# Attention, four experts and a SoLU layer: the experts' first layer as seven block products

## The chip, the cores and the metric

The kernel runs on one core of one Trainium2 chip. The time is the device time of one execution in microseconds, the median of several runs. TensorE (PE in the rows; PEld is its weight load), VectorE (DVE), ScalarE (ACT), GpSimd (POOL) and SyncE (SP, which issues most transfers) work side by side and wait for one another through semaphores.

## What is computed

```python
a = attention(q, k, v)            # 2 x 8 heads, 768 rows, 64 wide: 8 first keys and a band of 96
x = a as rows                     # 1536 x 512
p = probs / (probs.sum(-1) + 1e-9)
for e in range(4):                # w1[e] 512 x 1024, w2[e] 1024 x 512
    h = np.maximum(x @ w1[e], 0.0)
    out += p[:, e:e+1] * (h @ w2[e])
h = out @ w_in                    # 512 x 1024
solu = h * softmax(h)
ln = (solu - mean) / sqrt(var + 1e-6) * g_ln
return ln @ w_out                 # 1536 x 512
```

Everything is float32. The matmuls of the experts and of the last layer run in the format fp32r, in which TensorE takes one pass, but with fewer bits; so each operand is split into `hi` (the rounded value) and `lo` (what is left), and a product is three matmuls into one sum: hi·hi, hi·lo, lo·hi. ScalarE and GpSimd make the `hi` parts by a copy into fp32r, VectorE and GpSimd the `lo` parts by a subtraction.

## The kernel before

The program has three stages.

**Attention.** Heads go two at a time, eight pairs, each in three steps of 128 x 2 rows; `j` counts rounds of two pairs, six steps b = 0 to 5. In one step TensorE does `scores(b)`, `turn(b-1)` (transposes of the exponentials) and `values(b-2)`; VectorE adds the bias and takes row maxima (`add_bias`, L1034), ScalarE the exponentials (L830); both copy transposes out of PSUM (L840, L1043). After a pair VectorE normalises it (L1050 to L1056), TensorE transposes it (`turn_pair`, L623), ScalarE writes `xT_hi` (L846) and VectorE `xT_lo` (L1064). GpSimd meanwhile builds the values' windows (`copy_windows`, L480), the biases (`scale_bias`) and expert 0's first-layer weights (`split_w1`, L455 and L457).

**Experts.** The 1536 tokens go in three groups of 512, for four experts: `STEPS` = 12 steps n of eight chunks c of 128 hidden columns. `hidden(n, c)` (L569) computes one chunk, transposed, for 512 tokens: 4 slices of x by 3 matmuls, w stationary, x streaming 512 columns. ScalarE's `relu_hi` (L825) and VectorE's `relu_lo` (L1014) turn the bank in PSUM into h_hi and h_lo. `mix(n, c)` (L690) multiplies four token tiles of them, stationary, with the chunk's rows of w2, 512 columns streaming, into four banks `y_ps` that collect all eight chunks. `hidden` is three chunks ahead of `mix`:

```python
with pe.Fori(0, STEPS - 1) as n:
    for c in range(FC):
        hidden(n, c + AHEAD) ...   # or hidden(n + 1, c + AHEAD - FC)
        mix(n, c)
```

At the end of a step VectorE's `add_up` (L1172, L1174) adds the four banks, weighted with the expert's probability, to `acc`. GpSimd splits the next expert's weights chunk by chunk as the old ones come free (L461, L463).

**Last layer.** Twelve tiles s of 128 tokens: VectorE stages rows of `acc` (`stage`, L1195), TensorE transposes them (`turn_x`, L701) and multiplies with w_in (`up`, L743); `norm` on VectorE (L1219 to L1248) with ScalarE's exponential and one small power on GpSimd (L553); then `turn_ln` (L755) and `down` (L765) with w_out, which GpSimd has scaled by the gain (L542) and split. w_in's `hi` part is ScalarE's (L911) and its `lo` part VectorE's (L1257).

Each engine has its own program; the order of work is written out by hand, and is what the loops give.

## Time and profile before

| what | value |
|---|---|
| median of 3 runs (lowest, highest) | 793.17 us (793.15, 794.11) |
| the profiled execution | 793.0 us |
| its span, first to last instruction | 791.1 us |
| TensorE busy, matmuls | 786.6 us, 3838 |
| VectorE, ScalarE, GpSimd busy | 263.6, 164.2, 169.0 us |
| moved by DMA | 36.98 MB |

1.9 us of the profiled execution lie outside its span. The page's first part gives each engine's busy time, its second the span in 40 slices; a matmul's busy time in a row runs from its start to the modelled end of its pipeline, so that neighbours overlap, and how long one holds TensorE is read from starts, or from the chain of waits, which counts each piece up to the next one. A weight load overlaps with the matmul before it.

### The profile page before, as it was taken

How to read it: one execution, taken by the hardware profiler on the slowest of the kernel's cores; microseconds unless marked ns; L12 is line 12 of the kernel's file. 1: busy time of each engine (PE TensorE's matmuls, PEld its weight loads, DVE VectorE, ACT ScalarE, POOL GpSimd, SP SyncE). 2: the span in 40 equal slices, each digit the busy share in tenths (PEclk: the TensorE clock that was granted, in tenths of full speed). 3: DMA queues.
4: the chain of work that ended last, by engine and by line, in shares of the span. 5: the costliest groups of instructions: out<-in, count | busy, mean ns of one | idle time of the engine just before them, and what ended most of it. 6: DMA issues, size and time to landing. Idle time of an engine off the chain costs nothing.

```text
span 791.1 us, 11238 instructions
## 1 busy us (share of the span) xinstructions
PE 786.6 (99%) x3838; PEld 642.1 (81%) x3838; DVE 263.6 (33%) x586; ACT 164.2 (21%) x301; POOL 169.0 (21%) x221
## 2 busy tenths in 40 slices
PE   9999999999999999999999999999999999999998
PEld 8888888888888888888888888888888888888886
DVE  5676621211212121211212121211214268565653
ACT  4666511110101010101010111101011213222222
POOL 5334530000562000066000016620001320000000
PEclk9999999999999999999999999999999999999999
DMA  9744730000005000000500000130000000000001
GB/s 264 197 129 138 232 108 1 0 0 0 0 0 212 0 0 0 0 0 0 212 0 0 0 0 0 62 150 0 0 0 1 0 1 14 27 13 27 14 27 40
DMA packets 34133, 36.98 MB, mean 47 GB/s; under 512 B 14145, under 2 KB 25409, under 8 KB 34113
## 3 DMA queue, kind: packets, MB, share of 16 engines
q1 hardware_dynamic: 32000, 34.64, 13.8%
q10 hardware_dynamic: 2112, 2.10, 0.8%
q8 instruction: 10, 0.16, 0.1%
q14 instruction: 11, 0.08, 0.0%
HBM read 33.59 MB, written 3.15 MB: 46 GB/s over the span
## 4 chain that ended last, share of the span: by engine, by line
PE 95%; issue 4%; DVE 0%; POOL 0%; ACT 0%; POOLq 0%
PE y_ps L690 34%; PE h_ps L569 34%; PE out_ps L765 7%; PE h_ps L743 6%; PE o_ps L613 5%; PE s_ps L586 3%; PE pT_ps L596 3%; PE lnT_ps L755 1%; PE h_ps L765 1%; PE xt_ps L623 1%; PE o_ps L707 1%; PE xr_ps L701 0%; PE o_ps L630 0%; POOL stats L553 0%; DVE ln_lo L1205 0%
## 5 line engine op out<-in xcount | busy, mean ns | idle before, releaser
L1014 DVE SCALAR_TENSOR_TENSOR h_lo<-h_ps,h_hi 128x512 fp32r<-128x512 f32 x96 | 66.4, 692 | 403.7 <-ACT h_hi L825 403.7
L825 ACT ACTIVATE h_hi<-h_ps 128x512 fp32r<-128x512 f32 x96 | 57.5, 599 | 467.8 <-PE h_ps L569 467.8
L690 PE MATMUL y_ps<-w_hi,h_hi 128*128 128x512 f32 x384 | 153.2, 399 | 0.0
L690 PE MATMUL y_ps<-w_hi,h_lo 128*128 128x512 f32 x384 | 152.0, 396 | 0.0
L569 PE MATMUL h_ps<-xT_lo,w_hi 128*128 (+1 forms) x384 | 151.9, 396 | 0.0
L569 PE MATMUL h_ps<-xT_hi,w_hi 128*128 (+1 forms) x384 | 151.9, 396 | 0.0
L690 PE MATMUL y_ps<-w_lo,h_hi 128*128 128x512 f32 x384 | 151.7, 395 | 0.0
L569 PE MATMUL h_ps<-xT_hi,w_lo 128*128 (+1 forms) x384 | 151.5, 395 | 0.0
L690 PEld LDWEIGHTS y_ps<-w_hi,h_lo 128*128 128x128 f32 x384 | 72.5, 189 | 18.5
L569 PEld LDWEIGHTS h_ps<-xT_hi,w_hi 128*128 128x128 f32 x384 | 72.1, 188 | 17.8
L690 PEld LDWEIGHTS y_ps<-w_lo,h_hi 128*128 128x128 f32 x384 | 72.1, 188 | 17.4
L569 PEld LDWEIGHTS h_ps<-xT_hi,w_lo 128*128 128x128 f32 x384 | 72.1, 188 | 17.4
L569 PEld LDWEIGHTS h_ps<-xT_lo,w_hi 128*128 128x128 f32 x384 | 72.2, 188 | 17.0
L690 PEld LDWEIGHTS y_ps<-w_hi,h_hi 128*128 128x128 f32 x384 | 72.1, 188 | 16.7
L455 POOL CAST w_hi<-w_raw 128x512 fp32r<-128x512 f32 (+1 forms) x32 | 19.6, 612 | 228.1 <-PE h_ps L569 224.8
L461 POOL CAST w_hi<-w_raw 128x512 fp32r<-128x512 f32 x40 | 24.5, 612 | 188.2 <-issue 95.5
L463 POOL TENSOR_TENSOR w_lo<-w_raw,w_hi 128x512 fp32r<-128x512 f32 x40 | 51.9, 1298 | 3.2
L830 ACT ACTIVATE neg_s<-neg_s,row 128x256 f32<-128x256 f32 (+1 forms) x96 | 42.4, 482 | 26.1 <-DVE row L1034 25.9
L457 POOL TENSOR_TENSOR w_lo<-w_raw,w_hi 128x512 fp32r<-128x512 f32 (+1 forms) x32 | 41.4, 1293 | 2.9 <-POOL w_hi L455 0.7
L613 PE MATMUL o_ps<-v_sb,pT 128*128 128x65 f32 x352 | 42.0, 271 | 0.0
L1034 DVE CUSTOM_DVE_ANT_0 neg_s<-s_ps,bias 128x256 f32<-128x256 f32 (+1 forms) x96 | 34.4, 399 | 21.1 <-PE s_ps L586 18.8
L613 PEld LDWEIGHTS o_ps<-v_sb,pT 128*128 128x128 f32 x352 | 41.3, 192 | 0.1
(98 smaller groups left out, 771.0 us busy)
## 6 DMA issues: line engine op xcount, KB each, us to landing
w_raw<-in_w SPq DMA_DIRECT2D x7, 2048.0 KB, 9.8
qk<-in_qkW SPq DMA_DIRECT2D x24, 256.0 KB, 3.9
...
```

What stands on the lines that cost most here:

```text
L457: nc.gpsimd.tensor_tensor(lo, part, f32(hi), ALU.subtract).then_inc(w1_ready, 1)
L461: nc.gpsimd.tensor_copy(w2_hi[:, c], w2_raw[:, c]).then_inc(w2_hi_ready, 1)
L463: nc.gpsimd.tensor_tensor(w2_lo[:, c], w2_raw[:, c], f32(w2_hi[:, c]), ALU.subtract).then_inc(w2_ready, 1)
L569: mm = nc.tensor.matmul(h_ps[c % H_RING][:, :], w[:, c, k, :], x[:, k, cols], start=(k == 0 and x is xT_hi and w is w1_hi), stop=(k == KC ...
L613: mm = nc.tensor.matmul(o_ps[:, m, i * DV:(i + 1) * DV], pT[:, c % 2, e, (2 * m + half) * P:(2 * m + half + 1) * P], v_sb[:, p, m, at, :], ...
L690: mm = nc.tensor.matmul(y_ps[t][:, :], h[:, c % H_RING, tok], w[:, c, :], start=(c == 0 and h is h_hi and w is w2_hi), stop=(c == FC - 1 a ...
L743: mm = nc.tensor.matmul(h2_ps[m][:, b * HALF:(b + 1) * HALF], x[:, m, k, :], w[:, b * FC // 2:(b + 1) * FC // 2, k, :], start=(k == 0 and ...
L765: mm = nc.tensor.matmul(out_at(s), x[:, m, c, :], w[:, c, :], start=(c == 0 and x is ln_hi and w is w2_hi), stop=(c == FC - 1 and x is ln_lo))
L825: nc.scalar.activation(h_hi[:, c % H_RING, :], h_ps[c % H_RING][:, :], ACT.Relu).then_inc(hhi_ready, 1)
L830: nc.scalar.activation(tile, tile, ACT.Exp, bias=row[:, b // STEPS_PAIR, m, i:i + 1], scale=-1.0).then_inc(exp_ready, 1)
L1014: nc.vector.scalar_tensor_tensor(h_lo[:, c % H_RING, :], h_ps[c % H_RING][:, :], 0.0, f32(h_hi[:, c % H_RING, :]), ALU.max, ALU.subtract). ...
L1034: nc.vector.tensor_tensor_reduce(o, s, c, -SCALE, 3e38, ALU.add, ALU.min, row[:, b // STEPS_PAIR, m, i:i + 1]).then_inc(biased, 1)
```

## The change

The product of one weight block and x is done by Strassen's algorithm, in the form with 15 additions. A step is now 2 chunks (256 hidden columns) of one expert for one batch of 768 tokens. Both are halved three times over: the contraction of 512 in pairs of 128-slices, the 256 hidden columns in two chunks, the 768 tokens in two halves of `NB` = 384. Eight block products of 2 slices each become seven, on seven blocks of weights and seven of x, of which four each are sums of others:

- `ws[slot]`: the seven weight blocks, hi and lo, of a group g of two chunks (16 groups, two slots). GpSimd makes them: `weigh_sums` and `weigh_parts`; `split_w2` splits the group's two chunks of w2.
- `xs`: the seven blocks of x for both batches, made once, in the attention stage. VectorE makes the sums (`even_sums`, `odd_sums`, `odd_rest`), ScalarE the hi parts (`even_hi`, `odd_hi`, `sum_hi`), GpSimd the lo parts of the four sums (`x_lo`).
- `product(s, n, ...)` on TensorE: two slices by three matmuls of 384 columns into one of four banks `p_ps`; seven of them a step, in the order 1, 2, 6, 7, 5, 3, 4, in 16 x 2 = 32 steps s.
- ScalarE copies product 1 to SBUF (`keep`); seven additions of VectorE on 384 columns combine the products into four blocks of h in SBUF (`first_block` to `lower_block`); `relu_hi` and `relu_lo` split each into `hs`, reading it from SBUF.
- `mix(s, t, ...)`: six token tiles a step, each the sum over the step's two chunks only (6 matmuls of 512 columns), in one of three banks; `add_up` adds each of them to `acc`, six times a step.

The mixes of a step lie between the products of the next one. Weights come in transfers of 512 KB a group instead of 2048 KB an expert. w_in and w_out are loaded near the end, and GpSimd alone splits both. The large tensors are laid out anew in SBUF; attention and last layer compute as before. The cut diff:

```diff
-    GT = 4
-    GW = GT * P
-    NG = T // GW
-    STEPS = E * NG
+    NB = S // 2
+    SETS = 7
+    BLOCKS = 4
+    GROUPS = E * FC // 2
+    STEPS = GROUPS * B
+    TILES = QB
+    Y_BANKS = 3
+    ORDER = (1, 2, 6, 7, 5, 3, 4)
+    LAST = STEPS - 1
...
+            def load_weights(g):
+
+                e, q, slot = g // (FC // 2), g % (FC // 2), g % 2
+                sp.wait_ge(w1_ready, g - 1)
+                sp.dma_start(raw[:, slot, :].rearrange("p (k f) -> p k f", k=KC),
+                             w1[e].rearrange("(k p) f -> p k f", p=P)[:, :, 2 * P * q:2 * P * (q + 1)]
+                             ).then_inc(w1_loaded[slot], 16)
+                sp.wait_ge(w2_ready, g - 1)
+                sp.dma_start(raw[:, 2 + slot, :].rearrange("p (f n) -> p f n", f=2),
+                             w2[e].rearrange("(c p) n -> p c n", p=P)[:, 2 * q:2 * q + 2, :]
+                             ).then_inc(w2_loaded[slot], 16)
...
+                nc.gpsimd.tensor_tensor(sum_[:, 4], part(0, 1, slot), part(1, 1, slot), ALU.add).then_inc(w1_step, 1)
+                nc.gpsimd.tensor_tensor(sum_[:, 6], part(0, 0, slot), part(0, 1, slot), ALU.subtract).then_inc(w1_step, 1)
...
+                nc.gpsimd.tensor_copy(hi[:, 3:7], sum_[:, 3:7]).then_inc(w1_step, 1)
...
+                nc.gpsimd.tensor_tensor(lo[:, 3:7], sum_[:, 3:7], f32(hi[:, 3:7]), ALU.subtract).then_inc(w1_ready, 1)
...
+            def x_lo(j):
+
+                pool.wait_ge(xs_sum, START + 6 * j + 5)
+                for n, i in enumerate((5, 6, 4, 2)):
+                    pool.wait_ge(xs_hi, START + 7 * j + 3 + n + 1)
+                    pool.sem_inc(pool_waited, 1)
+                    nc.gpsimd.tensor_tensor(xs[:, j, 0, i], xs_sum_sb[:, j, 0, i], f32(xs[:, j, 1, i]), ALU.subtract
+                                            ).then_inc(xs_lo, 1)
...
+            with pool.Fori(1, GROUPS // 2) as a:
+                for slot in range(2):
+                    weigh_sums(2 * a + slot, slot)
+                    weigh_parts(2 * a + slot, slot)
+                    split_w2(2 * a + slot, slot)
+
+            pool.wait_ge(win_loaded, 16)
+            pool.wait_ge(p_done, SETS * LAST)
             for c in range(FC):
-                split_w2(0, c)
-            with pool.Fori(1, E) as e:
-                pool.wait_ge(w1_loaded, FIRST + 16 * e)
-                pool.wait_ge(w2_loaded, 16 * e + 16)
-                for c in range(FC):
-
-                    pool.wait_ge(h_ready, FC * NG * e - FC + c + 1)
-                    split_w1(e, c)
-                    pool.wait_ge(h_used, H_RING + FC * NG * e - FC + c + 1)
-                    split_w2(e, c)
-
-            pool.wait_ge(w2_loaded, 16 * E + 16)
+                part_c = raw[:, :, c * P:(c + 1) * P]
+                pool.sem_inc(pool_waited, 1)
+                nc.gpsimd.tensor_copy(win_hi[:, c], part_c).then_inc(win_step, 1)
+                pool.wait_ge(win_step, c + 1)
+                pool.sem_inc(pool_waited, 1)
+                nc.gpsimd.tensor_tensor(win_lo[:, c], part_c, f32(win_hi[:, c]), ALU.subtract).then_inc(win_ready, 1)
...
-            def hidden(n, c, chunks=range(KC)):
...
-                for k in chunks:
-                    for w, x in ((w1_hi, xT_hi), (w1_hi, xT_lo), (w1_lo, xT_hi)):
-                        mm = nc.tensor.matmul(h_ps[c % H_RING][:, :], w[:, c, k, :], x[:, k, cols],
-                                              start=(k == 0 and x is xT_hi and w is w1_hi),
...
+            def product(s, n, i, g):
+
...
+                if n == 1:
+                    pe.wait_ge(w1_ready, g + 1)
+                    at_least(pe, p_sum, SETS * s - 4)
+                if n == 2:
+                    at_least(pe, p_sum, SETS * s - 2)
+                if n == 6:
+                    at_least(pe, p_sum, SETS * s - 1)
+                if n == 7:
+                    at_least(pe, p_sum, SETS * s)
+                if n == 5:
+                    pe.wait_ge(p_kept, s + 1)
+                if n == 3:
+                    pe.wait_ge(p_sum, SETS * s + 1)
+                if n == 4:
+                    pe.wait_ge(p_sum, SETS * s + 2)
...
+                for kk in range(2):
+                    for w, x in ((1, 1), (1, 0), (0, 1)):
+                        mm = nc.tensor.matmul(bank, ws[slot][:, w, part, kk, :], xs[:, 2 * bt + kk, x, part, :],
+                                              start=(kk == 0 and w == 1 and x == 1),
+                                              stop=(kk == 1 and w == 0))
+                mm.then_inc(p_done, 1)
+
+            def mix(s, t, slot, bt, g):
+
+                if t == 0:
+                    pe.wait_ge(w2_ready, g + 1)
+                    pe.wait_ge(h_split, BLOCKS * s + BLOCKS)
+                at_least(pe, acc_written, TILES * s + t + 1 - Y_BANKS)
+                tok = slice((t % 3) * P, (t % 3 + 1) * P)
+                for f in range(2):
+                    b = 2 * f + t // 3
+                    for h, w in ((1, 1), (1, 0), (0, 1)):
+                        mm = nc.tensor.matmul(y_ps[t % Y_BANKS][:, :], hs[bt][:, h, b, tok], w2s[slot][:, w, f, :],
+                                              start=(f == 0 and h == 1 and w == 1), stop=(f == 1 and h == 0))
+                mm.then_inc(y_done, 1)
...
-                pe.wait_ge(x_ready, START + HP)
-                hidden(0, 0)
+                pe.wait_ge(xs_sum, START + 12)
+                pe.wait_ge(xs_lo, START + 8)
+                product(0, 1, 0, 0)
+                product(0, 2, 0, 0)
                 values(OUTER, -1)
-                hidden(0, 1)
+                product(0, 6, 0, 0)
+                product(0, 7, 0, 0)
                 turn_pair(OUTER, -1)
-                hidden(0, 2)
+                for n in (5, 3, 4):
+                    product(0, n, 0, 0)
+
...
-            with pe.Fori(0, STEPS - 1) as n:
-                for c in range(FC):
-                    if c + AHEAD < FC:
-                        hidden(n, c + AHEAD)
-                    else:
-                        hidden(n + 1, c + AHEAD - FC)
-                    if c == 0:
-                        pe.wait_ge(x_ready, START + R)
-                    mix(n, c)
...
+            def step(a, i):
+
+                s, g, last = 4 * a + i, 2 * a + i // 2, 4 * a + i - 1
+                last_slot, last_bt, last_g = (i - 1) // 2 % 2, (i - 1) % 2, 2 * a + (i - 1) // 2
+                new = isinstance(a, int) and s == 1
+                if new:
+                    pe.wait_ge(xs_sum, START + 19)
+                product(s, 1, i, g)
+                if new:
+                    pe.wait_ge(xs_sum, START + 24)
+                product(s, 2, i, g)
+                mix(last, 0, last_slot, last_bt, last_g)
+                if new:
+                    pe.wait_ge(xs_lo, START + 13)
...
+                product(s, 7, i, g)
...
+                product(s, 5, i, g)
...
+            def relu_hi(s, b, bt):
+
+                act.wait_ge(p_sum, SETS * s + {0: 1, 3: 4, 1: 6, 2: 7}[b])
+                nc.scalar.activation(hs[bt][:, 1, b], hs_sum[bt][:, 0, b], ACT.Relu).then_inc(hhi_ready, 1)
...
-            def relu_lo(n, c):
-                dve.wait_ge(hhi_ready, FC * n + c + 1)
-                nc.vector.scalar_tensor_tensor(h_lo[:, c % H_RING, :], h_ps[c % H_RING][:, :], 0.0,
-                                               f32(h_hi[:, c % H_RING, :]), ALU.max, ALU.subtract
...
+            def first_block(s, i):
+
+                dve.wait_ge(p_done, SETS * s + 2)
+                dve.wait_ge(p_kept, s + 1)
+                at_least(dve, y_done, TILES * (s - 1))
+                nc.vector.tensor_tensor(hs_sum[i % 2][:, 0, 0], p_bank(i, 2), kept[:, 0, :], ALU.add).then_inc(p_sum, 1)
...
+            def last_block(s, i):
+                dve.wait_ge(p_done, SETS * s + 5)
+                dve.wait_ge(p_sum, SETS * s + 3)
+                nc.vector.tensor_tensor(hs_sum[i % 2][:, 0, 3], p_bank(i, 5), kept[:, 2, :], ALU.add).then_inc(p_sum, 1)
...
+
+            def lower_block(s, i):
+                dve.wait_ge(p_done, SETS * s + 7)
+                nc.vector.tensor_tensor(hs_sum[i % 2][:, 0, 2], p_bank(i, 4), kept[:, 2, :], ALU.add).then_inc(p_sum, 1)
...
+            def relu_lo(s, b, bt):
+
+                dve.wait_ge(hhi_ready, BLOCKS * s + {0: 1, 3: 2, 1: 3, 2: 4}[b])
+                nc.vector.scalar_tensor_tensor(hs[bt][:, 0, b], hs_sum[bt][:, 0, b], 0.0, f32(hs[bt][:, 1, b]), ALU.max, ALU.subtract
                                                ).then_inc(h_split, 1)
...
+            def halve(a, i):
+
...
+                first_block(s, i)
+                add_up(s - 1, 0, 1 - bt, expert, first)
+                relu_lo(s, 0, bt)
+                second_sum(s, i)
+                third_sum(s, i)
+                add_up(s - 1, 1, 1 - bt, expert, first)
+                last_block(s, i)
+                fourth_sum(s, i)
+                add_up(s - 1, 2, 1 - bt, expert, first)
+                relu_lo(s, 3, bt)
+                right_block(s, i)
+                add_up(s - 1, 3, 1 - bt, expert, first)
+                relu_lo(s, 1, bt)
+                lower_block(s, i)
+                add_up(s - 1, 4, 1 - bt, expert, first)
+                relu_lo(s, 2, bt)
+                add_up(s - 1, 5, 1 - bt, expert, first)
```

On TensorE in the expert stage, the loop's body before; `h_ps` is a chunk's bank, `y_ps` a token tile's, rows without a tile prepare waits:

```order
L569 REGISTER_ALU
L569 MATMUL h_ps<-xT_lo,w_hi 128x512
L569 MATMUL h_ps<-xT_hi,w_lo 128x512
L682 REGISTER_ALU
L683 REGISTER_ALU
L687 ISA
L690 MATMUL y_ps<-w_hi,h_hi 128x512
L690 MATMUL y_ps<-w_lo,h_hi 128x512
L690 MATMUL y_ps<-w_hi,h_lo 128x512
```

and of the change, at the start of the loop's body (`p_ps` a product's bank, L48 and L702 the counters for semaphores):

```order
L48 ISA
L693 MATMUL p_ps<-xs,ws 128x384 x6
L48 REGISTER_ALU
L693 MATMUL p_ps<-xs,ws 128x384 x6
L702 ISA
L48 ISA
L708 MATMUL y_ps<-w2s,hs 128x512 x6
L48 REGISTER_ALU
L693 MATMUL p_ps<-xs,ws 128x384 x12
L48 REGISTER_ALU
L708 MATMUL y_ps<-w2s,hs 128x512 x6
```

Twelve matmuls of 512 columns in a chunk have become six of 384 in a product, and `mix` of the step before stands behind products 2, 7, 5, 3 and twice behind 4.

On VectorE where attention ends, before (`x_pair` is the last pair normalised, `xT_lo` its part of x):

```order
L1043 COPY pT<-pT_ps 128x512
L1064 TENSOR_TENSOR xT_lo<-xt_ps,xT_hi 128x768
L1014 SCALAR_TENSOR_TENSOR h_lo<-h_ps,h_hi 128x512
L1050 TENSOR_SCALAR sums<-o_ps 128x12
L1052 RECIPROCAL sums<-sums 128x12
L1056 TENSOR_TENSOR x_pair<-o_ps,sums 128x2x6x64
L1014 SCALAR_TENSOR_TENSOR h_lo<-h_ps,h_hi 128x512
L1064 TENSOR_TENSOR xT_lo<-xt_ps,xT_hi 128x768
```

and of the change, from the third sum of step 0 on (L1223; `kept` and `hs_sum` are sums of products, `hs` the lo part of h, `xs` and `xs_sum` blocks of x):

```order
L1223 TENSOR_TENSOR kept<-p_ps,kept 128x384
L1316 TENSOR_TENSOR xs_sum<-xt_ps,xs_sum 128x384
L1317 TENSOR_TENSOR xs_sum<-xt_ps,xs_sum 128x384
L1228 TENSOR_TENSOR hs_sum<-p_ps,kept 128x384
L1323 TENSOR_TENSOR xs_sum<-xt_ps,xs_sum 128x384
L1324 TENSOR_TENSOR xs<-xt_ps,xs 128x2x384
L1231 TENSOR_TENSOR hs_sum<-p_ps,kept 128x384
L1246 SCALAR_TENSOR_TENSOR hs<-hs_sum,hs 128x384
L1236 TENSOR_TENSOR hs_sum<-p_ps,hs_sum 128x384
L1246 SCALAR_TENSOR_TENSOR hs<-hs_sum,hs 128x384
L1241 TENSOR_TENSOR hs_sum<-p_ps,kept 128x384
L1246 SCALAR_TENSOR_TENSOR hs<-hs_sum,hs 128x384
```

The x of the last pair is now four sums and one subtraction, between the additions of step 0's products, and all of step 0's four `relu_lo` (L1246) stand here.

## Rows read from the trace of the kernel before

**Rows 1.** The page: TensorE busy, and its granted clock in 40 slices.
```profile
PE 786.6 (99%) x3838; PEld 642.1 (81%) x3838; DVE 263.6 (33%) x586; ACT 164.2 (21%) x301; POOL 169.0 (21%) x221
PEclk9999999999999999999999999999999999999999
```

**Rows 2.** The page's chain that ended last, by engine and by line.
```profile
PE 95%; issue 4%; DVE 0%; POOL 0%; ACT 0%; POOLq 0%
PE y_ps L690 34%; PE h_ps L569 34%; PE out_ps L765 7%; PE h_ps L743 6%; PE o_ps L613 5%; PE s_ps L586 3%; PE pT_ps L596 3%; PE lnT_ps L755 1%; PE h_ps L765 1%; PE xt_ps L623 1%; PE o_ps L707 1%; PE xr_ps L701 0%; PE o_ps L630 0%; POOL stats L553 0%; DVE ln_lo L1205 0%
```

**Rows 3.** Waits of TensorE: for whom, us in total, times, longest.
```profile
PE o_ps L707 <- POOL pT L420: 1.0, 1, 1.0
```

**Rows 4.** Busy times (with instructions) in attention and in the experts' stage.
```profile
0.00:96.10 96.10, 95.11 (x791) 83.94 (x792) 61.86 (x248) 60.43 (x136) 41.85 (x80) 1.00 0.69 198
96.10:637.70 541.60, 541.60 (x2337) 436.35 (x2336) 107.69 (x159) 64.17 (x108) 118.58 (x128) 1.00 0.08 27
```

**Rows 5.** The chain in order of time: start, us, what. Pieces of many alike.
```profile
99.17 1.73 PE o_ps L613 x16
...
300.61 2.81 PE y_ps L690 x12
303.43 2.79 PE h_ps L569 x12
```

**Rows 6.** Single instructions in order of time: start us, busy us, engine, line.
```profile
96.12 0.19 PEld L569 LDWEIGHTS h_ps<-xT_hi,w_hi 128*128 128x128 f32 x1
96.23 0.19 PEld L569 LDWEIGHTS h_ps<-xT_lo,w_hi 128*128 128x128 f32 x1
...
300.45 0.40 PE L690 MATMUL y_ps<-w_hi,h_hi 128*128 128x512 f32 x1
300.45 0.19 PEld L690 LDWEIGHTS y_ps<-w_lo,h_hi 128*128 128x128 f32 x1
...
300.69 0.39 PE L690 MATMUL y_ps<-w_lo,h_hi 128*128 128x512 f32 x1
```

**Rows 7.** Groups of weight loads: busy us, mean ns of one, idle before.
```profile
L569 PEld LDWEIGHTS h_ps<-xT_hi,w_hi 128*128 128x128 f32 x384 | 72.1, 188 | 17.8
...
L613 PEld LDWEIGHTS o_ps<-v_sb,pT 128*128 128x128 f32 x352 | 41.3, 192 | 0.1
```

**Rows 8.** Groups of the other engines: busy us, mean ns | idle before, releaser.
```profile
L1014 DVE SCALAR_TENSOR_TENSOR h_lo<-h_ps,h_hi 128x512 fp32r<-128x512 f32 x96 | 66.4, 692 | 403.7 <-ACT h_hi L825 403.7
L1174 DVE SCALAR_TENSOR_TENSOR acc<-y_ps,pr,acc 128x512 f32 x32 | 21.8, 745 | 16.1 <-PE y_ps L690 16.1
L1064 DVE TENSOR_TENSOR xT_lo<-xt_ps,xT_hi 128x768 f32 x6 | 5.7, 948 | 0.0
L825 ACT ACTIVATE h_hi<-h_ps 128x512 fp32r<-128x512 f32 x96 | 57.5, 599 | 467.8 <-PE h_ps L569 467.8
L846 ACT ACTIVATE xT_hi<-xt_ps 128x768 f32 x6 | 4.9, 815 | 2.2 <-PE xt_ps L623 2.2
L461 POOL CAST w_hi<-w_raw 128x512 fp32r<-128x512 f32 x40 | 24.5, 612 | 188.2 <-issue 95.5 <-PE y_ps L690 88.4 <-DMA w_raw<-in_w 4.2
L463 POOL TENSOR_TENSOR w_lo<-w_raw,w_hi 128x512 fp32r<-128x512 f32 x40 | 51.9, 1298 | 3.2
L542 POOL TENSOR_SCALAR w_raw<-w_raw,gain_sb 128x512 f32<-128x512 f32 x8 | 5.4, 699 | 9.8 <-DMA w_raw<-in_w_out 9.8
```

**Rows 9.** Attention, instructions of last round; in brackets idle before.
```profile
82.55 0.73 POOL L480 COPY v_sb<-v_sb 128x650 f32<-128x650 f32 x1 [6.28 <-DMA v_sb<-in_v]
...
89.78 0.17 DVE L1050 TENSOR_SCALAR sums<-o_ps 128x12 f32<-128x12 f32 x1 [0.83 <-PE o_ps L613]
...
91.57 0.91 ACT L830 ACTIVATE neg_s<-neg_s,row 128x256 f32<-128x256 f32 x2 [1.18 <-DVE row L1034]
```

**Rows 10.** First `up`, first power on GpSimd, first `turn_ln`, in order of time.
```profile
637.73 0.40 PE L743 MATMUL h_ps<-w_hi,x_hi 128*128 128x512 f32 x1
...
649.74 0.57 POOL L553 TENSOR_TENSOR stats<-stats,minus_half 128x1 f32<-128x1 f32 x1 [9.70 <-DVE stats L1241]
...
652.64 1.03 PE L755 MATMUL lnT_ps<-ident,solu 128*128 128x128 f32 x8
```

More of the change, by code:

```diff
@@ L45, in freed, with at_least @@
     return START + u + 1 - ring
+def at_least(eng, semaphore, value):
+    if not isinstance(value, int) or value > 0:
+        eng.wait_ge(semaphore, value)
 def f32(ap):
@@ L539, in _ @@
-            pool.wait_ge(w2_loaded, 16 * E + 16)
+                weigh_sums(0, 0)
+                weigh_parts(0, 0)
+                split_w2(0, 0)
+                for j in range(OUTER - 1):
+                    x_lo(j)
+            x_lo(OUTER - 1)
+            weigh_sums(1, 1)
+            weigh_parts(1, 1)
+            split_w2(1, 1)
+            with pool.Fori(1, GROUPS // 2) as a:
[3 more added lines that the diff above has]
+                    split_w2(2 * a + slot, slot)
@@ L736, in up @@
+            for i in range(1, 4):
+                step(0, i)
+            with pe.Fori(1, STEPS // 4) as a:
+                for i in range(4):
+                    step(a, i)
+            for t in range(TILES):
+                mix(LAST, t, 1, 1, GROUPS - 1)
+                if t in (1, 3):
+                    turn_x(t // 2, t // 2)
             def up(s, m, b):
@@ L1177, in mix_step, with halve @@
-            def mix_step(n, first=False):
-                for c in range(AHEAD, FC):
-                    relu_lo(n, c)
-                for c in range(AHEAD):
-                    relu_lo(n + 1, c)
-                add_up(n, first)
-            for c in range(EARLY, AHEAD):
-                relu_lo(0, c)
-            with dve.Fori(0, NG) as n:
-                mix_step(n, first=True)
-            with dve.Fori(NG, STEPS - 1) as n:
-                mix_step(n)
+            def halve(a, i):
+                s, bt = 4 * a + i, i % 2
+                first = isinstance(a, int) and s <= 2
+                expert = a // 2 if i else (a - 1) // 2
+                first_block(s, i)
[15 more added lines that the diff above has]
+                add_up(s - 1, 5, 1 - bt, expert, first)
```

584 lines of the change are left out of this document (356 added, 228 removed).

## The prediction, made before the changed kernel ran

> **What bounds the kernel now.** I read the page's first part, its slices and its chain of waits, then the waits of TensorE alone, the busy times by stage, and single instructions. TensorE is busy for 786.6 of 791.1 us, and the granted clock is at its upper level, 2.4 GHz, in all 40 slices (the 9s of PEclk) [rows 1]; the chain that ended last is TensorE for 95%, and its two expert layers are 34% each [rows 2]. The longest wait of TensorE for another engine is 1.0 us, at the very start [rows 3]. Attention takes the first 96.1 us, the experts 541.6 us, in which VectorE is busy 107.7, ScalarE 64.2 and GpSimd 118.6 us [rows 4]; the last stage takes the rest. So the time is TensorE's own stream, and what decides is the duration of one matmul with its weight load, not any wait.
>
> In the expert stage twelve first-layer matmuls (`hidden`) take 2.79 us in the chain, 0.2327 us each, and twelve of the second layer (`mix`) 2.81 us, 0.2342 each [rows 5]. A busy duration of 0.39 to 0.40 in a matmul's row is not its price, since the next one starts after 0.23 [rows 6]. 512 columns at 2.4 GHz are 213.3 ns; 19.4 ns are left over per matmul of `hidden`. What the 19.4 ns hang on is the question of this change.
>
> **First layer.** Before: 12 steps x 8 chunks x 12 = 1152 matmuls of 512 columns, x 0.2327 = 268.1 us. After: 32 steps x 7 products x 6 = 1344 matmuls of 384 columns: 516 thousand columns for 590 thousand (7/8), but 192 matmuls more. I take the 19.4 ns as a cost of each matmul, whatever its width: 160.0 + 19.4 = 179.4 ns, and 1344 x 0.1794 = 241.1 us. **Gain 27.0 us.** Bounds: the stream alone, 160.0 ns, gives 215.0 us (gain 53). Upwards, a weight load's row lasts 188 ns [rows 7] and starts with the matmul before it, both at 300.45 [rows 6]; were the next matmul to wait for the end of that record and the left-over 19.4 ns, one would cost 207.6 ns, 279.0 us in all (loss 11); if it stayed at 0.2327, 312.7 us (loss 45). I choose 179.4 because the record of a load overstates it: sixteen matmuls of 65 columns, each with a load of 192 ns by its row [rows 7], take 1.73 us, 0.108 each [rows 5], and the first two loads of `hidden` start 0.11 us apart, at 96.12 and 96.23 [rows 6]. A load thus fits in 160 ns.
>
> The Trainium skill (TensorE: Matmul & The Clock Gate, "Wait — 56ns, not 53.3ns?") says that warm back-to-back matmuls cost N/2.4 plus a fixed 2.5 ns or so. By that the trace's 512 columns would take 215.8 ns and not 232.7, so its figure isn't this kernel's; with its 162.5 ns the first layer would fall to 218.4 us, an estimate by that page. That the extra is fixed per matmul is what I too assume.
>
> **Second layer.** 32 x 6 x 2 x 3 = 1152 matmuls of 512 columns as before, 0. The additions to `acc` go from 48 to 192 on VectorE.
>
> **Cover in a steady step.** A step is 42 x 0.1794 + 36 x 0.2342 = 16.0 us of TensorE. VectorE's 384-column operations cost 0.56 us (from 0.692 at 512 and 0.948 at 768 [rows 8]): seven sums and four `relu_lo`, 6.2 us, and six `add_up` at 0.745, 4.5 us: 10.7 of 16.0. ScalarE: five at 0.49 (between 0.599 at 512 and 0.815 at 768 [rows 8]), 2.5. GpSimd per weight group, that is per two steps: 3840 columns of additions and subtractions at 1.298 us per 512, 9.7 us, and 2816 of casts at 0.612, 3.4 us [rows 8]: 13.1 of 31.9. All fit. The tightest wait is `mix(s,0)` for all four blocks of the step before. From the end of product 4 TensorE has two mixes and products 1 and 2 to do, 2.81 + 2.15 = 4.96 us; behind product 4 VectorE does `lower_block`, then `add_up(4)`, which itself waits 1.4 us for its mix, then `relu_lo`: about 0.2 + 1.4 + 0.75 + 0.56 = 2.9 us. Margin 2 us; ScalarE's `relu_hi` runs under it. Banks: products have four banks, three mixes are in flight, and each is asked for again at least two products later. Steady cost 0.
>
> **Attention.** x's blocks cost ScalarE four more copies of 384 columns per two pairs, and VectorE 1.5 us more at step b=4. VectorE idled 0.83 us and ScalarE 1.18 us before the operations next in line there [rows 9]; about 0.5 us of lateness is left, for TensorE 0 to 1 us per round of j. GpSimd's `x_lo`, 4 x 0.97 = 3.9 us, takes the place of two `split_w1` of 1.91. I take 1 us in all, range 0 to 3. `copy_windows` sits behind `x_lo` in GpSimd's queue, where GpSimd idled 6.28 us for v's load [rows 9]: hidden.
>
> **Turn from attention to the experts.** New wait. Before, `hidden` followed without a gap. Now, after the last pair is turned, TensorE has products 5, 3, 4 of step 0 and 1, 2 of step 1, 5.4 us, and then needs `mix(0,0)`, with no earlier mixes as cover. In that time: ScalarE's copy of the odd pair 0.8, ten 384-column operations of VectorE in a row at about 0.5 (they overlap by 0.08), a 768-column one 0.9, two waits for ScalarE's `relu_hi` 1.1, handovers 0.2: 8.0 us. **Stall 2.6 us**, range 1 to 5. Next late: `weigh_sums(1)` and `weigh_parts(1)`, 9.3 us on GpSimd, begin about 1 us after `mix(0,0)` and are needed 13.8 us after it: 3.5 us of margin.
>
> **Turn to the last stage.** GpSimd alone now splits w_in and w_out: 8 x 1.91, 8 x 0.70, 8 x 1.91 = 36.2 us, from the end of step 30's products, before it may give norm 0 its power. Before, that came 12.0 us after the first `up`, at 649.74 after 637.73 [rows 10]. Available: 2.8 (two mixes of step 30) + 16.0 (step 31) + 8.4 (its mixes) + 0.9 (two `turn_x`) + 12.0 = 40.1 us; the transposes that need the result come 2.9 us after it [rows 10]. Cost 0, range 0 to 3. w_in itself needs 15.3 of 28 us. The loads are issued 20 us or more ahead.
>
> **Sum**, against the profiled execution: span 791.1 - 27.0 + 2.6 + 1.0 = 767.7 us; 1.9 us lie around the span (793.0 in all), so 769.6. The median of the runs is 793.17, so I leave it there: **769.6 us.** No change means within 0.2%, 1.6 us, about what a measurement can tell.
>
> **Rivals.**
> 1. *The left-over goes with the columns* (0.2327 x 3/4 = 0.1745 us). For it: 19.4 ns is unlike any other row's remainder. Against: nothing in the trace has another width in this number format. 1344 x 0.1745 = 234.5, 763 us. Chance 0.12. The same kind, further: it belongs to a full bank of 512 columns and is gone at 384, 160.0 ns; 791.1 - 53.1 + 3.6 + 1.9 = 743.5 us, chance 0.02, since nothing speaks for it but the lack of a narrow row. The skill's 2.5 ns, above, would come out close to it, at 746.9 us.
> 2. *VectorE blocked by GpSimd.* `relu_lo` now reads both inputs from SBUF (h was in PSUM). Should it wait for one whole 1024-column subtraction of GpSimd, 2 x 1.298 = 2.6 us [rows 8], the 2.9 us become 5.5, 0.5 over the cover; in every one of 31 steps 16 us, 785 us. Against it: GpSimd is busy 41% of a step, and mostly elsewhere than behind product 4. Chance 0.06. The Trainium skill (SBUF — State Buffer, "Who interferes with whom") says that a VectorE instruction with two SBUF inputs contends with a GpSimd instruction that reads SBUF; in before's expert stage VectorE read one input from PSUM, so no row here shows it.
> 3. *Slower: the load record counts* (207.6 ns per product, above). 791.1 + 10.9 + 3.6 + 1.9 = 807.5 us. It decides from (268.1 - 3.6)/1344 = 196.8 ns per narrow matmul upwards: there the seven products cost what the eight did. Against: the 0.108 us of rows 5. Chance 0.05.
> 4. *Several stalls longer than counted* (a late weight group, a half clock after the 2.6 us gap, GpSimd late for norm 0), 775 to 782 us. Chance 0.07.
>
> **How the numbers follow.** Forecast 0.68, rivals 0.12 and 0.02, 0.06, 0.05, 0.07. The range takes in the forecast with its stalls at both ends (766 to 775), rival 1 and rival 4: 761 to 781; rivals 2 and 3 and a share of the others stay out. Faster by over 0.2%: all but rival 3 and 0.03 out of rival 4 for stalls beyond those named, 0.92; within it 0.02; slower 0.06.
>
> **What would show it.** In the profile after: twelve `p_ps` matmuls in 2.15 us (2.09 under rival 1, 2.5 under rival 3), six `y_ps` in 1.41; a step of 16.0 us; one TensorE wait of 2 to 3 us for `hs` at about 110 us and hardly another; `up` beginning near 614 us, which is 637.7 - 27.0 + 3.6. Wrong would be waits of TensorE for VectorE or for `ws` in every step, or narrow matmuls over 190 ns apart.

## The result, and the profile after

The changed kernel takes **763.48 us** (median of 4 runs, 762.55 to 763.95), the kernel before 793.32 us beside it: a ratio of 0.9621, 95% interval 0.9604 to 0.9637. That is 3.8% faster. The forecast was 769.6 us; the gain is 29.8 us where it said 23.6. The profiled execution is the fastest of the four (762.55 us, span 760.8 us); the others, 763.4 to 764.0, show a granted clock of 0.996 on average where it shows 0.998.

The page, TensorE and the others, against [rows 1]:

```profile
PE 752.5 (99%) x4030; PEld 661.7 (87%) x4030; DVE 493.9 (65%) x994; ACT 191.5 (25%) x377; POOL 288.5 (38%) x317
```

TensorE is still the bound. VectorE went from 33 to 65% of the span. The waits of TensorE, against [rows 3] (for whom, us in total, times, longest):

```profile
PE y_ps L708 <- DVE hs L1246: 3.2, 1, 3.2
PE o_ps L825 <- POOL pT L477: 1.0, 1, 1.0
PE out_ps L915 <- DVE ln_lo L1491: 0.5, 1, 0.5
PE p_ps L693 <- DVE hs_sum L1231: 0.2, 1, 0.2
```

One new wait of 3.2 us, and none that comes back in every step. The busy times by stage, against [rows 4] (attention, then the experts up to the first `up`):

```profile
0.00:96.10 96.10, 95.10 (x783) 83.43 (x783) 65.06 (x260) 64.14 (x151) 44.09 (x80) 1.00 0.58 165
96.10:608.60 512.50, 509.09 (x2538) 456.38 (x2537) 335.62 (x557) 87.77 (x170) 226.72 (x215) 1.00 0.11 35
```

The experts' stage went from 541.6 to 512.5 us. The chain in order of time, one step of the new stage (start, us, what), against [rows 5]:

```profile
300.84 2.08 PE p_ps L693 x12
302.93 1.39 PE y_ps L708 x6
304.31 2.11 PE p_ps L693 x12
306.42 1.39 PE y_ps L708 x6
307.81 1.06 PE p_ps L693 x6
...
313.77 2.79 PE y_ps L708 x12
316.56 0.52 PE p_ps L693 x3
```

A step lasts 316.56 - 300.84 = 15.72 us, TensorE without a gap: 42 narrow matmuls in 7.37 us (2.08, 2.11 and three times 1.06), 0.1755 each, and 36 wide ones in 8.35 us, 0.232 each. The other steps last 15.64 to 15.75 us. Averaged over the steps between 130 and 600 us, a narrow matmul starts 0.1746 us before the next one and a wide one 0.2329. Forecast were 0.1794, 0.2342 and 16.0 us.

The turn from attention to the experts, in order of time (start, busy us, engine, line, in brackets the idle time before and its releaser):

```profile
107.04 1.99 POOL L562 TENSOR_TENSOR xs<-xs_sum,xs 128x384 fp32r<-128x384 f32 x2 [9.49 <-DVE xs_sum L1323]
107.61 0.55 DVE L1231 TENSOR_TENSOR hs_sum<-p_ps,kept 128x384 f32<-128x384 f32 x1
108.08 1.36 DVE L1246 SCALAR_TENSOR_TENSOR hs<-hs_sum,hs 128x384 fp32r<-128x384 f32 x1
...
108.31 1.28 PE L693 MATMUL p_ps<-xs,ws 128*128 128x384 f32 x6 [0.19 <-DVE hs_sum L1231]
109.36 0.55 DVE L1236 TENSOR_TENSOR hs_sum<-p_ps,hs_sum 128x384 f32<-128x384 f32 x1
...
110.49 0.56 DVE L1246 SCALAR_TENSOR_TENSOR hs<-hs_sum,hs 128x384 fp32r<-128x384 f32 x1 [0.59 <-ACT hs L982]
...
112.10 0.56 DVE L1246 SCALAR_TENSOR_TENSOR hs<-hs_sum,hs 128x384 fp32r<-128x384 f32 x1 [0.59 <-ACT hs L982]
...
112.81 2.90 PE L708 MATMUL y_ps<-w2s,hs 128*128 128x512 f32 x6 [3.22 <-DVE hs L1246]
```

Three things are to be seen. VectorE works from 107.61 to 112.66 with two pauses of 0.59 us, both for ScalarE's `relu_hi`, and TensorE waits for its last `relu_lo`. The first `relu_lo`, two inputs from SBUF, takes 1.36 us in place of 0.56 while GpSimd's `x_lo` runs (107.04 to 109.03). And the six matmuls of the first mix take 2.90 us, not 1.62 by the same count. Two windows, over the end of the wait and over the mix, show why (length, busy times, then the granted clock, 0.57 and 0.50):

```profile
112.30:112.80 0.50, 0.00 (x0) 0.02 (x1) 0.36 (x1) 0.50 (x2) 0.14 (x1) 0.57 0.06 16
112.80:115.50 2.70, 2.69 (x6) 2.13 (x7) 0.56 (x1) 0.58 (x2) 2.70 (x4) 0.50 0.01 3
```

The clock fell while TensorE still waited, and stayed at 1.2 GHz until about 115.8 us (from there to 117.0 it is 1.00 again); that costs 1.3 us.

The last stage, GpSimd's first and last split and its first power, against [rows 10]:

```profile
580.96 0.63 POOL L641 CAST win_hi<-raw 128x512 fp32r<-128x512 f32 x1 [24.90 <-PE p_ps L693]
...
619.46 1.29 POOL L657 TENSOR_TENSOR wout_lo<-wout_lo_sum,wout_hi_b 128x512 fp32r<-128x512 f32 x1 [0.18 <-POOL wout_hi_b L654]
620.75 0.57 POOL L664 TENSOR_TENSOR stats<-stats,minus_half 128x1 f32<-128x1 f32 x1
```

The first `up` starts at 608.66, and the power 12.1 us later: before it was 12.0. GpSimd came to it straight from its splits, with no idle time left (9.70 us of it in [rows 10]); the value that the power needs had been ready for 0.1 us.

### The profile page after: what moved, and what is told of

Same layout as the page of the kernel before. It is cut to its first block, busy times and chain, and to the rows that moved or that the text cites. A ratio compares the mean times of both kernels' runs of the same rounds, so it can differ in the third digit from the quotient of the medians.

```text
span 760.8 us, 12768 instructions
## 1 busy us (share of the span) xinstructions
PE 752.5 (99%) x4030; PEld 661.7 (87%) x4030; DVE 493.9 (65%) x994; ACT 191.5 (25%) x377; POOL 288.5 (38%) x317
## 4 chain that ended last, share of the span: by engine, by line
PE 76%; issue 17%; POOL 5%; DVE 1%; ACT 0%; POOLq 0%; DVEq 0%
PE y_ps L708 33%; PE p_ps L693 29%; PE o_ps L749 5%; PE s_ps L722 3%; PE pT_ps L732 3%; POOL win_lo L644 1%; POOL wout_lo L657 1%; PE o_ps L825 1%; PE xt_ps L760 1%; POOL wout_lo_sum L649 1%; POOL win_hi L641 1%; POOL stats L664 1%; POOL wout_hi_b L654 0%; PE o_ps L767 0%; PE out_ps L917 0%
## 5 line engine op out<-in xcount | busy, mean ns | idle before, releaser
L708 PE MATMUL y_ps<-w2s,hs 128*128 128x512 f32 x1152 | 295.3, 396 | 3.2 <-DVE hs L1246 3.2
L693 PE MATMUL p_ps<-xs,ws 128*128 128x384 f32 x1344 | 260.7, 337 | 0.2 <-DVE hs_sum L1231 0.2
L693 PEld LDWEIGHTS p_ps<-xs,ws 128*128 128x128 f32 x1344 | 239.0, 188 | 14.3 <-issue 0.5
L708 PEld LDWEIGHTS y_ps<-w2s,hs 128*128 128x128 f32 x1152 | 215.0, 189 | 41.5 <-issue 3.9
L1259 DVE SCALAR_TENSOR_TENSOR acc<-y_ps,pr,acc 128x512 f32<-128x512 f32 x180 | 135.1, 750 | 108.0 <-PE y_ps L708 107.9
L982 ACT ACTIVATE hs<-hs_sum 128x384 fp32r<-128x384 f32 x128 | 67.3, 526 | 330.9 <-DVE hs_sum L1228 164.4
L1246 DVE SCALAR_TENSOR_TENSOR hs<-hs_sum,hs 128x384 fp32r<-128x384 f32 x128 | 82.6, 645 | 1.8 <-ACT hs L982 1.8
L520 POOL TENSOR_TENSOR ws_sum<-raw 128x256 f32<-128x256 f32 x16 | 12.2, 759 | 122.2 <-PE p_ps L693 121.6
L543 POOL TENSOR_TENSOR ws<-ws_sum,ws 128x1024 fp32r<-128x1024 f32 x16 | 39.5, 2470 | 2.9 <-POOL ws L540 2.9
L554 POOL TENSOR_TENSOR w2s<-raw,w2s 128x1024 fp32r<-128x1024 f32 x16 | 38.9, 2432 | 2.9 <-POOL w2s L551 2.9
L894 PE MATMUL h_ps<-win_hi,x_hi 128*128 128x512 f32 x96 | 38.9, 405 | 0.0
```

Of the source, the lines that this page charges most:

```text
L543: nc.gpsimd.tensor_tensor(lo[:, 3:7], sum_[:, 3:7], f32(hi[:, 3:7]), ALU.subtract).then_inc(w1_ready, 1)
L554: nc.gpsimd.tensor_tensor(lo, rows, f32(hi), ALU.subtract).then_inc(w2_ready, 1)
L693: mm = nc.tensor.matmul(bank, ws[slot][:, w, part, kk, :], xs[:, 2 * bt + kk, x, part, :], start=(kk == 0 and w == 1 and x == 1), stop=(kk ...
L708: mm = nc.tensor.matmul(y_ps[t % Y_BANKS][:, :], hs[bt][:, h, b, tok], w2s[slot][:, w, f, :], start=(f == 0 and h == 1 and w == 1), stop=( ...
L894: mm = nc.tensor.matmul(h2_ps[m][:, b * HALF:(b + 1) * HALF], x[:, m, k, :], w[:, b * FC // 2:(b + 1) * FC // 2, k, :], start=(k == 0 and ...
L982: nc.scalar.activation(hs[bt][:, 1, b], hs_sum[bt][:, 0, b], ACT.Relu).then_inc(hhi_ready, 1)
```

## The experiments

Twelve kernels. Two questions: what does the time beyond the columns hang on (the term that was furthest off), and what makes up the turn and the margins that the sum set at nothing?

### 1 to 3. Narrower first-layer matmuls in the kernel before

```
-  cols = bass.ds((n % NG) * GW, GW)
   for k in chunks:
       for w, x in ((w1_hi, xT_hi), (w1_hi, xT_lo), (w1_lo, xT_hi)):
+          width = GW if (k == 0 and x is xT_hi and w is w1_hi) else 384   # or 256, 128
+          cols = bass.ds((n % NG) * GW, width)
```

> The kernel before, in which 11 of the 12 matmuls of each of the first layer's 96 chunks take only 384 of their 512 columns (the first, which starts the sum, keeps 512; so part of the hidden activations is missing from the sums). 1056 matmuls are narrowed. Theory A, the time beyond the columns grows with the columns: 233.0 ns x 384/512 = 174.8 ns from start to start, 61.4 us saved, about 732 us. Theory B, the 19.4 ns are fixed per matmul (the forecast): 179.4 ns, 56.6 us saved, about 737 us. Theory C, the price belongs to the change's other order of products and not to the width: neither, a figure apart from the 174.9 ns that the changed kernel shows.

> As the run at 384 columns, now 256 of 512 (the rest of the sums is left out). Theory A: 116.5 ns from start to start, 123 us saved, about 670 us. Theory B: 106.7 + 19.4 = 126.1 ns, 113 us saved, about 680 us. Where a floor per matmul (its weight load) lies above 116.5 ns, both fail and the period is that floor.

> As the run at 384 columns, now 128 of 512. Theory A: 58.3 ns from start to start, 184 us saved, about 609 us. Theory B: 72.7 ns, 169 us saved, about 624 us. If a matmul that changes its weights costs at least its weight load, a floor that shows only below some width, the period stays at that floor (over 100 ns), at least 140 us saved but no more: 650 us or so. That would say how far a product could be narrowed before it stops paying.

Measured: 731.29, 671.92 and 665.98 us, one run each, before 793.45. From the chain, twelve matmuls of one chunk, of which the first has 512 columns (0.233 us). At 384, 256 and 128 columns:

```profile
304.07 2.15 PE h_ps L570 x12
```
```profile
303.29 1.53 PE h_ps L570 x12
```
```profile
304.54 1.41 PE h_ps L570 x12
```

The eleven narrow ones take (2.15 - 0.233)/11 = 0.174 us, 0.118 us and, by the same count, 0.107 us. At 384 columns that is the 0.1748 of theory A and what the changed kernel shows, and not the 0.1794 of theory B; theory C falls, since the order of the products isn't in this kernel. At 256 it is 0.118, by A 0.1165, by B 0.126. At 128 both fail, and single starts show that the average hides something: the first narrow matmul is followed after 0.06 us, the ten behind it come 0.11 us apart (1.11 us between the first two rows here), and the first mix holds TensorE for 0.28 us, where 0.23 is usual.

```profile
300.42 0.27 PE L570 MATMUL h_ps<-xT_hi,w_lo 128*128 x1
...
301.53 0.44 PE L691 MATMUL y_ps<-w_hi,h_hi 128*128 128x512 f32 x1
301.81 0.39 PE L691 MATMUL y_ps<-w_lo,h_hi 128*128 128x512 f32 x1
```

Over the whole trace the ten lie 0.112 us apart, and the time of the run says the same: 127.5 us saved by 1056 matmuls is 0.1207 each, from 0.2327 to 0.112. (The 140 us that were expected at least would have meant a floor of 0.100.) The sixteen matmuls of 65 columns in [rows 5] come 0.112 us apart too, all but the first; their average of 0.108 has the same short start in it. So a matmul with its own weights costs its columns x 0.455 ns, but not less than about 0.112 us. The floor lies under the 0.175 us of the products: seven of 384 columns pay in full. By these figures, products of half that width would not (0.087 by the columns).

### 4. Zeros for x

In the kernel before, both parts of x are zero for the experts:

```
-  xt_ps[:, 0:S], ACT.Copy
+  xt_ps[:, 0:S], ACT.Copy, scale=0.0
-  nc.vector.tensor_tensor(lo, xt_ps[:, 0:S], f32(hi), ALU.subtract)
+  nc.vector.tensor_tensor(lo, f32(hi), f32(hi), ALU.subtract)
```

> The kernel before, in which both parts of x that the experts read are zero (so all hidden activations are zero and only the last stage's inputs are unchanged in kind). If the 19.7 ns beyond 213.3 ns per 512-column matmul come from the numbers that are multiplied (the chip slowing the array under load), they go: about 2304 x 0.0197 = 45 us less, near 748 us. If they belong to the operation as it is (type, width), nothing changes: 793 us within 0.2%, still 233 ns apart.

Measured: 793.21 us beside 793.45, and in the chain

```profile
303.49 2.79 PE h_ps L569 x12
306.29 2.81 PE y_ps L690 x12
```

Not a hundredth of a microsecond changes in a group of twelve. The left-over doesn't come from the numbers that are multiplied.

### 5. Eight products again

```
-  for kk in range(2):
+  for kk in (range(2) if n != 4 else (0, 1, 0, 1)):
```

> The changed kernel with product 4 computed twice over (its six matmuls run again with the same operands, the first of them starting the sum anew, so nothing of the output changes): eight products again, with all the rest of the change in place. If TensorE alone sets the pace, 32 steps x 6 x 0.1749 us = 33.6 us more: 797.1 us. If the time were set by what VectorE, ScalarE or GpSimd add per step, less than 20 us more. If the longer way from product 4 to its block of hs makes mix(s, 0) wait as well, over 37 us. What then stands between this run and the kernel before (793.3 us) is the price of everything else in the change, near 4 us.

Measured: 796.02 us (795.86 to 796.19), before 793.38 beside it. That is 32.5 us over the median of the changed kernel and 33.3 over its profiled run, by 33.6 expected. Product 4, computed twice, is the group of twelve here:

```profile
303.71 1.04 PE p_ps L693 x6
...
308.60 2.08 PE p_ps L693 x12
310.69 2.81 PE y_ps L708 x12
```

A step now lasts 16.68 to 16.79 us, 1.05 more, which is six matmuls. TensorE alone sets the pace of the step, and one product less is worth its matmuls. Against the kernel before, the rest of the change (144 more `add_up`, the sums, the turn, the last stage) costs 2.6 us, all in all.

### 6 to 8. The turn: VectorE's order, TensorE's order, both

VectorE, in `attend`; the second edit is TensorE's, in `step`, where `new` is step 1:

```
   fourth_sum(0, 0)
-  relu_lo(0, 3, 0)
   right_block(0, 0)
-  relu_lo(0, 1, 0)
   lower_block(0, 0)
+  relu_lo(0, 3, 0)
+  relu_lo(0, 1, 0)
   relu_lo(0, 2, 0)
...
   product(s, 2, i, g)
-  mix(last, 0, last_slot, last_bt, last_g)
+  if not new:
+      mix(last, 0, last_slot, last_bt, last_g)
...
   product(s, 7, i, g)
+  if new:
+      mix(last, 0, last_slot, last_bt, last_g)
```

> The changed kernel with one edit in VectorE's program at the turn from attention to experts: right_block and lower_block of step 0 come ahead of relu_lo of blocks 3, 1 and 2 in place of between them. If the 3.2 us of TensorE's wait come from VectorE's chain (a relu_lo that took 1.36 us beside GpSimd's subtraction, and two waits of 0.59 us for ScalarE's relu_hi), the last relu_lo ends about 1.8 us sooner: 761.7 us; and if the shorter gap also spares TensorE the fall to 1.2 GHz behind it, 1.3 us more: 760.4 us. If the wait had another cause (ScalarE late, GpSimd's x parts), no change: 763.5 us.

Measured: 761.20 us (759.74 to 761.82), by the changed kernel's 763.48. TensorE, in order of time:

```profile
111.32 1.63 PE L708 MATMUL y_ps<-w2s,hs 128*128 128x512 f32 x6 [2.03 <-DVE hs L1246]
```

The wait shrank from 3.22 to 2.03 us: VectorE's order was part of it, 1.2 us and not 1.8. In this execution the first mix ran at the full clock (1.63 us for six). The five runs fall into two kinds: two of 759.74 and 759.89 with a mean granted clock of 1.000, three of 761.20 to 761.82 with 0.998. The two kinds lie about 1.4 us apart, as if the clock fell behind the gap of 2 us in some executions and not in others; only a trace of the first kind was kept, so that is not shown.

> The changed kernel with one edit in TensorE's program: in step 1 mix(0, 0) comes behind product 7 in place of behind product 2. Products 6 and 7 (2.1 us) then lie where TensorE waited, as far as lower_block frees product 7's bank: the 3.2 us shrink to about 1.0 us in pieces, 761.4 us; with the clock kept at 2.4 GHz 1.3 us more, 760.1 us. If the later mix delays the chain of step 1 in turn (its sums and its bank), the gain is given back: 763.5 us.

Measured: 759.03 us (758.97 to 759.54), 4.5 us less; expected were 3.4 at most. TensorE in order of time:

```profile
108.44 1.29 PE L693 MATMUL p_ps<-xs,ws 128*128 128x384 f32 x6 [0.19 <-DVE hs_sum L1234]
110.19 1.28 PE L693 MATMUL p_ps<-xs,ws 128*128 128x384 f32 x6 [0.46 <-DVE hs_sum L1239]
111.80 1.31 PE L693 MATMUL p_ps<-xs,ws 128*128 128x384 f32 x6 [0.33 <-DVE hs_sum L1244]
112.95 3.03 PE L708 MATMUL y_ps<-w2s,hs 128*128 128x512 f32 x12
```

Products 6 and 7 wait 0.46 and 0.33 us for the blocks that free their banks, and the first mix comes without a wait: 1.0 us in pieces, as worked out. The clock stays at its upper level. The extra 1.1 us over the expectation is taken up by run 9.

> Both edits together, the candidate for a version that beats both kernels: VectorE's sums of step 0 ahead of its relu_lo, and mix(0, 0) behind product 7. By the chain the last relu_lo ends at about 110.9 us and product 7 at 111.7 us, so no wait is left: 3.2 us and, with the clock kept, 1.3 us less, 759.0 us. If the clock falls there for another reason than the gap, 760.3 us. If the edits do the same work, no better than the better of them alone.

Measured: **757.80 us** (757.71 to 758.34), ratio to the kernel before 0.9552 (0.9539 to 0.9565). This version beats both kernels, the changed one by 5.7 us. That it lies 1.2 us under the expectation has the same reason as in the run before. The chain at the turn:

```profile
107.98 3.39 PE p_ps L693 x18
111.36 2.99 PE y_ps L708 x12
```

Products 2, 6 and 7 in a row, and then two mixes: no wait is left but the 0.2 us ahead of product 2.

### 9. The gap filled with idle work

```
   product(s, 2, i, g)
+  if new:
+      for _ in range(28):
+          nc.tensor.transpose(spare_ps[:, 0:P], ident[:, :], ident[:, :])
   mix(last, 0, last_slot, last_bt, last_g)
```

> The changed kernel with 28 transposes of the identity matrix, into a bank that nothing reads, where TensorE waits for hs at the turn (behind product 2 of step 1, ahead of mix(0, 0)). At 0.108 to 0.12 us each they last 3.0 to 3.4 us and so lie inside the 3.56 us between the last product and the first mix: they shorten nothing and can only keep the engine busy. If the first mix ran at 1.2 GHz because of the gap ahead of it, it now runs at 2.4 GHz, and the time falls by the 1.3 us of its six matmuls, perhaps 2: 761.5 to 762.2 us, with the granted clock of that stretch at 1.00. If the clock falls there for another reason (TensorE's load, the start of the experts), nothing changes: 763.5 us, clock 0.50 there.

Measured: 761.11 us (761.03 to 761.33), 2.4 us less than the changed kernel's median and 1.4 less than its profiled run. TensorE in order of time, and the granted clock over the filler and over the mix behind it:

```profile
109.43 3.22 PE L858 MATMUL spare_ps<-ident 128*128 128x128 f32 x28
112.82 1.62 PE L708 MATMUL y_ps<-w2s,hs 128*128 128x512 f32 x6 [0.17 <-DVE hs L1249]
```
```profile
109.30:112.70 3.40, 3.35 (x30) 3.07 (x28) 2.19 (x5) 2.08 (x5) 1.03 (x2) 1.00 0.02 5
112.70:117.00 4.30, 4.18 (x21) 3.87 (x22) 2.98 (x5) 0.70 (x2) 4.12 (x6) 1.00 0.01 4
```

The first mix starts at 112.82, where it started at 112.81: the transposes shorten nothing. But it now takes 1.62 us, not 2.90. So it was the idle time ahead of it that took the clock down, and the cost is 1.3 us in the execution that was profiled. In the usual ones, those with a mean clock of 0.996, it is about 2.4 us by the medians (763.48 - 761.11); none of their traces was kept. That accounts for the extra 1.1 us of the pe_order run: 2.2 us less of waiting and 2.4 of half clock are 4.6, measured were 4.5.

### 10 and 11. How much VectorE's cover in a step holds

To the version of run 8, ahead of the counted addition in `lower_block`:

```
+  for r in range(3):                                   # or 6
+      nc.vector.tensor_tensor(scratch[:, r, :], p_bank(i, 4), kept[:, 2, :], ALU.add)
```

> The version with both edits (757.8 us) and three additions more on VectorE in every step, ahead of lower_block (product 4 plus the kept sum, into memory that nothing reads; 0.48 us each one behind the other, 1.44 us a step). In the changed kernel's step at 300 us the last relu_lo ends at 316.80 us and mix(s, 0) starts at 318.5 us, and VectorE idled 0.77 us on the way. If the cover is what the trace shows, the additions push relu_lo by 1.44 - 0.77 = 0.7 us, inside the 1.7 us of margin: no change, 757.8 us within 1 us. If VectorE's chain already set the step, or if its blocks under GpSimd's work eat the margin, 0.7 us in each of 31 steps: 779 us.

Measured: 759.34 us (758.91 to 760.24), 1.5 us over run 8 (757.80), half a microsecond more than expected.

> The same with six additions (2.9 us a step). By the trace's margin relu_lo is pushed by 2.9 - 0.77 = 2.1 us against 1.7 us: 0.4 us of waiting for hs in each of 31 steps, 12 us more, near 770 us (763 to 785, as the wait moves the other sums too and short waits may fall together with GpSimd's work). Without any margin 2.1 to 2.9 us a step, 823 to 848 us. No change at all would say that the margin is wider than read.

Measured: 779.14 us (778.65 to 780.49), 21.3 us over run 8. The waits of TensorE, with three additions and with six:

```profile
PE y_ps L709 <- issue: 0.5, 1, 0.5
PE y_ps L709 <- DVE hs L1252: 0.4, 1, 0.4
```
```profile
PE y_ps L709 <- DVE hs L1252: 5.5, 13, 0.5
PE y_ps L709 <- POOL w2s L555: 3.8, 2, 2.2
PE y_ps L709 <- issue: 2.4, 1, 2.4
PE p_ps L694 <- DVE hs_sum L1247: 1.6, 1, 1.6
```

With three, the steps stay as they were (15.64 to 15.75 us), though VectorE does 1.44 us more in each. The 1.5 us lie at the two ends, where fewer products or mixes cover VectorE: the first two mixes start 1.2 us later, at 112.56 for 111.33 us, and the last step adds 0.6.

With six, the run is 9 us over the forecast, and the starts of the steps tell where. Twenty-seven of them, all but the first two and the last, are longer than in run 8 by 0.45 us on average, 12.2 us together: the 12 that the margin gave. (The list above counts only the longer waits, thirteen of them.) The other 9.5 us of the traced span lie at the ends: 2.5 at the turn, 4.3 in two waits for GpSimd's `w2s` at 129 and 147 us, whose chain goes back to the last `x_lo`, and 2.7 in the last step, whose first mix has no products ahead of it. So the margin of a steady step is 2.9 - 0.77 - 0.45 = 1.7 us of lateness, as it was read.

### 12. GpSimd later in the last stage

```
   if c < 2:
+      nc.gpsimd.tensor_tensor(wout_hi(c), wout_raw[:, c], wout_raw[:, c], ALU.subtract).then_inc(wout_step, 1)
```

(with a wait for it ahead of the cast, and the counts of `wout_step` moved on; on the version of run 8)

> The version with both edits and two subtractions more in GpSimd's last work, the split of w_out (1.3 us each and a wait of 0.18 us, 3.0 us together, into columns that are written over right behind). GpSimd's last split then ends 3.0 us later. In the version with both edits it ended just as norm 0's variance was ready, so if its margin is used up, norm 0's power, the turned norm and the first out product come 3.0 us later: 760.5 to 760.8 us. If there is still cover (TensorE has other work at that point), less: 757.8 us.

Measured: 760.44 us (760.07 to 760.67), 2.6 us over run 8. GpSimd's first power now starts at 618.83 where run 8 had it at 615.95, 2.9 us later, again straight behind the last split:

```profile
617.58 1.29 POOL L661 TENSOR_TENSOR wout_lo<-wout_lo_sum,wout_hi_b 128x512 fp32r<-128x512 f32 x1 [0.18 <-POOL wout_hi_b L658]
618.83 0.57 POOL L668 TENSOR_TENSOR stats<-stats,minus_half 128x1 f32<-128x1 f32 x1
```

Nearly all of it reaches the end. The margin of this turn, 3.9 us by the forecast's sum, is used up.

## Why the prediction was right, and where its terms were off

The direction, the size within one percent and the mechanism held: TensorE's stream sets the time and the change shortens it. The span was forecast at 767.7 us and is 760.8, 6.9 us less. By the prediction's own steps:

- **First layer, "I take the 19.4 ns as a cost of each matmul, whatever its width."** This step failed. In the profile the 384-column matmuls start 0.1746 us apart on average, not 0.1794: 42 x 32 x 0.0048 = 6.5 us less. Runs 1 to 3 show the law in place of it: the left-over goes with the columns, which was rival 1 (763 us, chance 0.12). Run 4 rules out the data. The fixed figure of 2.5 ns of the Trainium skill (TensorE: Matmul & The Clock Gate, "Wait — 56ns, not 53.3ns?") would give 162.5 ns, an estimate by that page; run 1 shows 174.
- **That a weight load fits in 160 ns** was right, and the row of 65-column matmuls was the one to go by: the floor of run 3, 0.112 us, is what those matmuls show one by one. Rival 3, by which the 188 ns record would count, is dead: those records still read 188 ns in the profile after, and the products' matmuls come every 0.175 us. (Its 207.6 ns should be 188 + 19.4 = 207.4, which changes nothing.)
- **Second layer, 0.** A mix matmul now takes 0.2329 us on average for 0.2342: 36 x 32 x 0.0013 = 1.5 us gained that no step foresaw. It also holds in the last stage (from the first `up` to the end 153.4 us before, 152.1 after, 1.2 us less though one wait grew by 0.3). It isn't the narrower neighbours: in run 1, with the old layout and a first layer of 384 columns, the wide ones keep their 0.2342, and in run 5 they take 0.2329. The matmuls are the same; their order and the place of their operands in memory are not. No run took that apart, so its cause stays open.
- **Cover in a steady step, 0.** Right: no wait comes back. VectorE was busy for 335.6 of 512.5 us, 65% (forecast 10.7 of 16.0, 67%). The margin of `mix(s,0)` was given as 2 us: `relu_lo` ends at 316.80 and product 2 at about 318.6, so 1.8, and run 11 gives 1.7.
- **Rival 2, VectorE blocked by GpSimd.** The blocking is real, its price in a step is nothing. The rows of the 128 `relu_lo` and of ScalarE's `relu_hi` (busy us, mean ns of one):

```profile
L1246 DVE SCALAR_TENSOR_TENSOR hs<-hs_sum,hs 128x384 fp32r<-128x384 f32 x128 | 82.6, 645 | 1.8 <-ACT hs L982 1.8
L982 ACT ACTIVATE hs<-hs_sum 128x384 fp32r<-128x384 f32 x128 | 67.3, 526 | 330.9 <-DVE hs_sum L1228 164.4 <-DVE hs_sum L1236 68.7 <-DVE hs_sum L1241 58.8
```

  645 ns on average; the 83 that overlap no GpSimd instruction take 546 to 557: 12 us over the kernel, nearly all under TensorE's work. The longest, 1.83 us, began 1.0 us into a 1024-column subtraction of 2.40 us. The rule of the Trainium skill (SBUF — State Buffer, "Who interferes with whom") that a VectorE instruction with two SBUF inputs contends with GpSimd's reads is what the trace shows here; the sums, one input of which is in PSUM, stay at 547 to 558 ns.
- **Attention, +1.0.** The first product starts at 97.07, the first `hidden` matmul did at 96.14: 0.9 us.
- **Turn from attention to the experts, "Stall 2.6 us".** The place and the releaser were right, the size short. The waits are 3.2 and 0.2 us, and the half clock adds 1.3 (in most runs 2.4): 4.7 us in the profiled run. This term was mis-sized as well. The sum of VectorE's chain left out the 0.8 us by which GpSimd's `x_lo` held the first `relu_lo`. The half clock stood under rival 4 only, and it belonged in the sum: the gap that brought it on was itself forecast.
- **Turn to the last stage, 0 to 3 us.** The cost is near 0, with nothing to spare: GpSimd worked from 580.96 to 620.75, 39.8 us and not 36.2. A pair of cast and subtraction takes 2.03 us, since a handover of 0.18 us lies between them; the 1.91 of the sum left it out, the scaling took 6.18 us for 5.6, and a few casts ran up to 1.01 us for 0.61. Run 12 shows what the next microsecond costs.

The sum again with the measured terms: 767.7 - 6.5 - 1.5 + 0.8 (longer wait) + 1.3 (clock) - 1.2 (last stage) - 0.1 (attention) = 760.5 us, and the span is 760.8.

Some of the agreement is luck. The forecast's own bounds, with its stalls at both ends, ended at 766 us; the measured 763.48 is in the range because that had been drawn down for rival 1, at a chance of 0.12. And that rival's figure of 763 comes as near as it does because what its sum lacks cancels: 2.7 us gained in the second layer and the last stage, 2.1 lost at the turn, in most runs 3.2.
